# The low-weight product of the last 64 inputs as 64-row matmuls in the two halves of the array, expert stage

## What is computed

```python
N, D, E, F = (1536, 320, 4, 1024)
p = domain_probs / (domain_probs.sum(-1, keepdims=True) + 1e-09)
for e in range(E):
    h = np.maximum(x @ w1[e], 0.0)
    out += p[:, e:e + 1] * (h @ w2[e])
```

## Time and profile before

| what | value |
|---|---|
| device time, median of 3 runs | 687.5 us (687.5 to 687.73) |
| span of the profiled execution | 690.6 us |
| PE busy | 659.7 us, 96% of the span, 3700 matmuls |
| PEld busy | 568.0 us |
| DVE busy | 345.4 us |
| ACT busy | 192.8 us |
| POOL busy | 158.0 us |
| mean granted TensorE clock | 0.948 of full speed |

### The profile page before, as it was taken

The page is one execution under the profiler, slowest core; times in us unless marked ns, Lnnn a source line. Parts: engine busy times, 40 slices in busy tenths (PEclk is TensorE's granted clock), DMA queues, the critical chain, the costliest instruction groups (busy, mean ns, idle before and its releaser), DMA issues.

```text
span 690.6 us, 9787 instructions
## 1 busy us (share of the span) xinstructions
PE 659.7 (96%) x3700; PEld 568.0 (82%) x3700; DVE 345.4 (50%) x577; ACT 192.8 (28%) x366; POOL 158.0 (23%) x85
## 2 busy tenths in 40 slices
PE   3898999999999999988999999999999999999998
PEld 1556668889788888777989889998988988999888
DVE  4478668667686675665443333333323333333332
ACT  3344345433463442422121211112102112111110
POOL 0346424212151131365422022220222000000000
PEclk9566589999999999998999999999999999999999
DMA  6764333302532000122301101111020000000012
GB/s 153 219 192 159 76 101 87 87 0 50 128 86 60 26 0 0 47 84 84 122 1 46 39 1 47 38 47 39 1 85 1 0 1 1 1 0 1 1 39 76
DMA packets 9620, 38.45 MB, mean 56 GB/s; under 512 B 1144, under 2 KB 3416, under 8 KB 8144
## 3 DMA queue, kind: packets, MB, share of 16 engines
q1 hardware_dynamic: 9584, 37.94, 18.6%
HBM read 35.78 MB, written 2.16 MB: 55 GB/s over the span
## 4 chain that ended last, share of the span: by engine, by line
PE 89%; DVE 6%; DMA 2%; issue 1%; ACT 1%; SPq 0%; ACTq 0%; DVEq 0%
PE bank L420 12%; PE bank L421 12%; PE bank L422 12%; PE bank L411 9%; PE bank L412 9%; PE bank L413 9%; PE bank L408 5%; PE bank L409 4%; PE bank L380 4%; PE bank L398 3%; DVE g_lo L219 2%; PE bank L357 2%; PE bank L349 2%; PE bank L370 2%; PE bank L363 2%; DVE gbuf L723 1%
## 5 line engine op out<-in xcount | busy, mean ns | idle before, releaser
L420 PE MATMUL bank<-dn_hi,g_lo 128*128 128x320 f32 x576 | 181.0, 314 | 7.4 <-DVE ysum L731 6.0
L422 PE MATMUL bank<-dn_hi,g_hi 128*128 128x320 f32 x576 | 179.0, 311 | 0.0
L421 PE MATMUL bank<-dn_lo,g_hi 128*128 128x320 f32 x576 | 178.9, 311 | 0.0
L635 ACT ACTIVATE g_hi<-bank 128x512 fp32r<-128x512 f32 x96 | 57.4, 598 | 274.0 <-PE bank L413 274.0
L809 DVE SCALAR_TENSOR_TENSOR g_lo<-bank,g_hi 128x512 fp32r<-128x512 f32 x96 | 66.3, 691 | 120.3 <-ACT g_hi L635 120.0
L420 PEld LDWEIGHTS bank<-dn_hi,g_lo 128*128 128x128 f32 x576 | 109.0, 189 | 10.9 <-DVE ysum L731 6.8
L411 PE MATMUL bank<-xT,up_hi 128*128 128x512 f32 (+1 forms) x288 | 112.6, 391 | 0.0
L412 PE MATMUL bank<-xT,up_lo 128*128 128x512 f32 (+1 forms) x288 | 112.5, 391 | 0.0
L413 PE MATMUL bank<-xT,up_hi 128*128 128x512 f32 (+1 forms) x288 | 112.4, 390 | 0.0
L421 PEld LDWEIGHTS bank<-dn_lo,g_hi 128*128 128x128 f32 x576 | 108.9, 189 | 1.1
L422 PEld LDWEIGHTS bank<-dn_hi,g_hi 128*128 128x128 f32 x576 | 109.0, 189 | 0.0
(11 more groups left out here) (122 smaller groups left out, 711.1 us busy)
## 6 DMA issues: line engine op xcount, KB each, us to landing
raw<-qk_d SPq DMA_DIRECT2D x12, 960.0 KB, 7.3
up_raw<-up_d SPq DMA_DIRECT2D x12, 768.0 KB, 5.2
dn_raw<-down_d SPq DMA_DIRECT2D x12, 640.0 KB, 4.0
kvo<-kvo_d SPq DMA_DIRECT2D x12, 488.0 KB, 3.6
out_d<-acc SPq DMA_DIRECT2D x2, 640.0 KB, 3.3
out_d<-acc SPq DMA_DIRECT2D x4, 160.0 KB, 1.8
scratch_d<-split SPq DMA_DIRECT2D x1, 192.0 KB, 8.2
consts<-consts_d SPq DMA_DIRECT2D x1, 145.0 KB, 2.5
```

The source lines that it names most:

```text
L420: mm(dst[:, 0:DM], g_lo[:, par, f, toks], dn_hi[s][:, f, :], start=f == 0, stop=False)
L421: mm(dst[:, 0:DM], g_hi[:, par, f, toks], dn_lo[s][:, f, :], start=False, stop=False)
L422: last = mm(dst[:, 0:DM], g_hi[:, par, f, toks], dn_hi[s][:, f, :], start=False, stop=f == NF - 1)
L635: go(g_hi[:, j % 2, f, :], UPB[f][:, :], ACT.Relu).then_inc(hi2_done, 1)
```

## The change

In the expert stage `up_tile` is replaced by two functions. `rest_tile` issues the `up_lo` product of the last 64 inputs as a matmul of 64 rows: for even f with rows 0 to 63 of `up_lo` and `xT`, for odd f with rows 64 to 127 of `up_lo` and a copy of the high part, `xrest`, which SP brings to these rows by DMA. `full_tile` issues the other seven matmuls. In each turn the four `rest_tile` come first, then the four `full_tile`. The product of low x low parts of the last 64, which L409 had added, is left out. `xrest` lies where `kvo`, the attention's input, was. The feed-forward stage keeps `up_tile`.

```diff
+        def copy_rest(g):
+            toks = slice(g * GT, (g + 1) * GT)
+            sp.wait_ge(x2hi_done, UPG * (g + 1))
+            sp.dma_start(xrest[ROW1:2 * ROW1, toks].bitcast(F32), xT[0:ROW1, 4, toks].bitcast(F32)).then_inc(x2_copied[g], 16)
+
+        sp.wait_ge(y_done, NU)
+        for g in range(NG - 1):
+            copy_rest(g)
         for h in range(HB1, NH):
             s = h % SLOTS
+            if h == 2 * HB1:
+                copy_rest(NG - 1)
...
+        def rest_tile(dst, s, f, g):
+            half = f % 2
+            rows, cols = slice(half * ROW1, (half + 1) * ROW1), slice(f * P, (f + 1) * P)
+            toks = slice(g * GT, (g + 1) * GT)
+            mm(dst[:, :], up_lo[s][rows, 2, cols], xrest[rows, toks] if half else xT[rows, 4, toks], start=True, stop=False)
+
+        def full_tile(dst, s, f, g):
+            cols, toks = slice(f * P, (f + 1) * P), slice(g * GT, (g + 1) * GT)
+            mm(dst[:, :], up_hi[s][:, 2, cols], xT[:, 4, toks], start=False, stop=False)
+            for k in range(2):
+                mm(dst[:, :], up_hi[s][:, k, cols], xT[:, 2 + k, toks], start=False, stop=False)
+                mm(dst[:, :], up_lo[s][:, k, cols], xT[:, k, toks], start=False, stop=False)
+                last = mm(dst[:, :], up_hi[s][:, k, cols], xT[:, k, toks], start=False, stop=k == 1)
+            return last
...
                     if j < NG:
                         pe.wait_ge(x2lo_done, UPG * (g + 1) + 1)
+                        pe.wait_ge(x2_copied[g], 16)
                     for f in range(NF):
                         if j == 0 and f == 0:
                             pe.wait_ge(g_done, NF * HB1 * NG)
...
                             pe.wait_ge(x2lo_done, NU + 1)
                         if j > 0:
                             pe.wait_ge(lo2_done, NF * (m - 1) + f + 1)
-                        up_tile(UPB[f], slot, f, g * GT).then_inc(up2_done, 1)
+                        rest_tile(UPB[f], slot, f, g)
+                    for f in range(NF):
+                        full_tile(UPB[f], slot, f, g).then_inc(up2_done, 1)
```

More of the change, by code:

```diff
@@ L40 @@
 V1 = D + 2
+ROW1 = DM - 2 * P
 ST = 3 * D
@@ L125, in build @@
     high, _, _ = sb("high", [ST, HALF, P], F32R)
-    kvo, _, _ = sb("kvo", [P, 2, 2 * DM + H * V1], F32)
+    kvo, _, kvo_at = sb("kvo", [P, 2, 2 * DM + H * V1], F32)
+    xrest, _, _ = sb("xrest", [P, NU * P], F32R, kvo_at)
     pT, _, _ = sb("pT", [P, 2, HALF * P], F32)
@@ L208, in build @@
     x2T_done, x2hi_done, x2lo_done = map(sem, ("x2T_done", "x2hi_done", "x2lo_done"))
+    x2_copied = [sem(f"x2_copied{g}") for g in range(NG)]
     up2_done, hi2_done, lo2_done, dn2_done, dn2_read = map(
```

## The result

Measured beside each other in 20 runs each, the changed kernel takes 693.68 us and the kernel before 689.27 us (medians). The ratio, which leaves out one slow run of the changed kernel (698.98 us), is 1.0056, 95% interval 1.0031 to 1.0081: slower by 2.1 to 5.6 us. It is not the quotient of the two medians, which is 1.0064. On the 687.5 us shown above that is 691.4 us; 691.9 was predicted, in a range of 685.0 to 696.0.

A forecast was written before the change was run, and what follows sets the result against it. PE's matmul stream was taken to bound the expert stage. Start 0.84, j = 1 twice 2.42 and 21 regular blocks 1.18 make +4.4 us: 687.5 + 4.4 = 691.9 us, range 685.0 to 696.0.

The forecast's parts named there:

- The change of row count: Each expert-stage block pays for entering and leaving the 64-row group: 0.195 + 0.21 = 0.405 us.
- The faster rival: 64-row matmuls in the expert blocks pay nothing for the change of rows: 682.8 us; chance 0.10.
- What a pair saves: In each group, the second matmul of a pair ends 0.105 us behind the first; a regular block loses 0.056 us.
- the rival of 689.7 us: Pairs in the 64-row groups run without distance, +2.2 us in all; chance 0.20.
- The waits at j = 1: In both passes the fourth 64-row matmul waits for its bank: 1.21 us a block, 2.42 us in all.
- The start: At the first expert block the fourth matmul waits for DVE's last low part: 0.84 us, once.
- No overlap: Rival: the two halves of a 64-row pair do not run side by side, +11.8 us, 699.3 us; chance 0.10.
- The clock: Rival: the stall at j = 1 lowers the clock once or twice, 693.6 or 695.3 us; chance 0.10.
- The copies and the SP queue: The copies into `xrest` were taken at nothing; without their cover PE would wait about 3 us once.

The follow-up runs named there:

- e2_same_half: The changed kernel with all four 64-row matmuls of a group in rows 0 to 63, so none can overlap; ratio 1.0160 to the kernel before.
- e3_group_128: The changed kernel's order and waits, but the four first matmuls of a block have 128 rows as before; ratio 1.0042 to the kernel before.
- e1_from_j2: The changed kernel with the old `up_tile` kept in turns j = 0 and j = 1 of each pass; ratio 0.9983 to the kernel before.
- e5_halves_in_turn: The changed kernel with the halves within a group ordered upper, upper, lower, lower; ratio 1.0051 to the kernel before.

## Why the prediction was right

**The change of row count** was the main term, read from 24-row and 40-row matmuls, and 64 rows pay the same: 0.19 us of idle time ahead of the group, whose first pair ends 0.20 us later than one matmul would, and 0.43 us in place of 0.227 for the first full matmul. 0.405 us a block was forecast; a regular turn of e2_same_half, which has this and no overlap, gives 0.43. The faster rival is out. The price at which a regular block would break even, 0.349 us in the prediction, was that of pairs at a distance; without distance it is 0.454, and so a block gains a little in spite of the price.

**What a pair saves** is the term that was mis-sized. I took 0.105 us as the distance of two loads, from two 40-row loads in one half of the array. That distance holds for the same half; loads of different halves start 0.00 us apart. A regular block gains 0.04 us instead of losing 0.056; the bound that I had put beside it was a gain of 0.049. The Trainium skill, TensorE: Matmul & The Clock Gate, under Measured speedup vs the span model, has about 4 ns a tile between the starts. The trace agrees: the starts of a pair stand 0.00 us apart. This moves the sum from +4.4 to +2.3 us; the trace shows +2.35. So what happened was the rival of 689.7 us, to which I gave 0.20, and not the forecast. That the forecast of 691.9 is nearer to the 691.4 of the ratio is luck as far as the traces show: the ratio is itself uncertain by 1.7 us either way, and the 1.5 us by which it exceeds the trace's difference are in no term of the prediction.

**The waits at j = 1** were forecast at 1.21 us each and measured at 1.20, the fourth matmul ending 2.07 us behind the natural start; in the trace it ends at 352.17, and the natural start was 350.10. **The start** was forecast at 0.84 us and measured at 0.84. e3_group_128 shows both stalls without a 64-row matmul, e1_from_j2 shows the kernel without them.

**No overlap** would have cost 11.8 us; e2_same_half, where there is none, measured 1.016, 11.0 us. **The clock** did not fall at j = 1 in any trace of the changed kernel. **The copies and the SP queue** cost PE nothing: no wait for `x2_copied` shows among its waits. The third copy was issued at 342.41 and took 2.2 us to land, at 344.6 where 346 was expected, 19 us before it is needed.

## What to carry to other kernels

Issuing small matmuls in two halves of the array saves a slot a pair, and changing to them and back costs 0.4 us a group with float32r weights: with 512 columns one pair a group lost 0.19 us, two gained 0.04, and a third would by this count bring another 0.227 (an estimate; no run had three). Such a group belongs behind work that hides its waits. When an order is changed so that several banks are needed at once, look for the one turn where the same banks were filled just before; each time it cost 1.2 us here, more than 20 regular turns gave back. And a difference of a few tenths of a per cent is to be read from the stage that was changed, since the time up to it differs by more from run to run.

## What the runs showed of the hardware that was not expected

Weight loads of the two halves start together (365.72 and 365.72 in the changed kernel), loads of the same half 0.10 us apart. A 64-row matmul of the free half starts 0.33 us ahead of its elder neighbour in the program (374.93 and 375.26 in e5_halves_in_turn). Between the two passes of a loop of 960 matmuls PE stood idle for 0.94 to 1.45 us or for 2.69 to 3.15, and not when the loop was written out; after the long kind the clock fell from 2.4 to 1.2 GHz, for 3.4 us in e3_group_128.
